# First products two units ahead of the second ones, w2's loads behind w1's, the second tile in halves, and a mixed last pair of units

## What is computed

```python
# x: [1536, 512] from the attention
logits = x @ w_gate                       # [1536, 8]
expert_idx = np.argmax(logits, axis=1)    # gate_w: softmax probability of that expert
for e in range(8):
    xe = x[expert_idx == e]
    h = np.maximum(xe @ w1[e], 0.0)       # w1[e]: [512, 1024]
    out[expert_idx == e] = gate_w * (h @ w2[e])   # w2[e]: [1024, 512]
h = out @ w_in                            # [512, 2048]
y = (h - np.tanh(h)) @ w_out              # [2048, 512]
```

## Time and profile before

| | us |
|---|---|
| median of 3 runs | 540.94 (538.23 to 541.13) |
| the profiled execution, its own time | 545.5 |
| its span, first to last instruction | 543.7 |
| TensorE busy | 516.3 (95%) |
| VectorE, ScalarE, GpSimd busy | 366.3, 262.3, 317.3 |
| mean granted clock of TensorE | 0.986 of 2.4 GHz |
| attention and routing | to about 73 |
| experts | about 73 to 270 |
| last stage and stores | about 270 to 543.7 |

### The profile page before, as it was taken

One profiled execution on the slowest core, in us unless ns is written; L12 is line 12 of the kernel. 1 busy time (PEld: TensorE's weight loads), 2 busy tenths in 40 slices (PEclk: granted clock), 3 DMA queues, 4 the chain that ended last, 5 costly groups with the idle time before them and its releaser, 6 DMA issues.

```text
span 543.7 us, 10934 instructions
## 1 busy us (share of the span) xinstructions
PE 516.3 (95%) x3974; PEld 458.5 (84%) x3975; DVE 366.3 (67%) x539; ACT 262.3 (48%) x484; POOL 317.3 (58%) x263
## 2 busy tenths in 40 slices
PE   5999959999899999999999999999999999999994
PEld 4999849999899999999878888888888888888883
DVE  7455444564436555365379999989997775997771
ACT  1244515655557666565455455545534444443431
POOL 4866056644344444454379898976855553875553
PEclk9999988999899999999999999999999999999998
DMA  8788636567576767766270000000100000100001
GB/s 321 249 287 287 202 115 186 205 196 204 181 222 203 230 184 224 243 184 214 89 276 1 1 1 1 1 1 25 54 1 1 0 1 1 59 20 2 0 1 77
DMA packets 32410, 64.56 MB, mean 119 GB/s; under 512 B 3696, under 2 KB 7792, under 8 KB 32368
## 3 DMA queue, kind: packets, MB, share of 16 engines
q1 hardware_dynamic: 30448, 57.71, 32.4%
q0 software_dynamic: 1920, 6.29, 3.5%
HBM read 57.69 MB, written 6.29 MB: 118 GB/s over the span
## 4 chain that ended last, share of the span: by engine, by line
PE 87%; DMA 4%; DVE 3%; issue 2%; ACT 2%; POOL 1%; SPq 1%; ACTq 0%; DVEq 0%; POOLq 0%
PE bank L315 26%; PE bank L317 25%; PE bank L316 25%; DMA wst<-in_w_dram 3%; PE bank L1129 2%; PE bank L1104 2%; PE bank L1115 2%; PE bank L1150 1%; PE bank L1212 1%; PE bank L1141 1%; PE bank L1157 1%; POOL out_dram L644 1%; DMA x_sorted<-token_rows,tokid 1%; ACT x_h L744 1%; PE bank L1287 1%
## 5 line engine op out<-in xcount | busy, mean ns | idle before, releaser
L603 POOL TENSOR_TENSOR w_l<-wst,w_h 128x512 fp32r<-128x512 f32 x64 | 84.0, 1313 | 93.6 <-ACT w_h L723 93.5
L652 POOL TENSOR_SCALAR big<-h_sq 128x512 uint8<-128x512 f32 x48 | 79.8, 1663 | 37.4 <-ACT h_sq L797 37.1
L665 POOL TENSOR_TENSOR g_l<-g,g_h 128x512 fp32r<-128x512 f32 x48 | 63.7, 1327 | 46.0 <-ACT g_h L807 46.0
L315 PE MATMUL bank<-xs_h,w_h 128*128 (+1 forms) x256 | 72.2, 282 | 4.2 <-DVE xs_l L1012 1.4
L315 PE MATMUL bank<-wo_h,g_h 128*128 128x512 f32 x192 | 75.4, 392 | 0.0
L317 PE MATMUL bank<-wo_l,g_h 128*128 128x512 f32 x192 | 75.1, 391 | 0.0
L316 PE MATMUL bank<-wo_h,g_l 128*128 128x512 f32 x192 | 74.6, 389 | 0.0
L317 PE MATMUL bank<-x_l,win_h 128*128 128x512 f32 x188 | 74.3, 395 | 0.0
L315 PE MATMUL bank<-h_h,w_h 128*128 128x232 f32 x256 | 71.9, 281 | 2.1 <-DVE h_l L1003 1.9
L315 PE MATMUL bank<-x_h,win_h 128*128 128x512 f32 x188 | 73.9, 393 | 0.0
L316 PE MATMUL bank<-x_h,win_l 128*128 128x512 f32 x188 | 73.7, 392 | 0.0
(11 more groups left out here) (146 smaller groups left out, 1111.0 us busy)
## 6 DMA issues: line engine op xcount, KB each, us to landing
wst<-in_w_dram SPq DMA_DIRECT2D x128, 256.0 KB, 3.1
qk_in<-in_qk_t_dram SPq DMA_DIRECT2D x12, 512.0 KB, 5.4
kv_in<-in_kv_dram SPq DMA_DIRECT2D x12, 512.0 KB, 4.5
win<-in_w_in_dram SPq DMA_DIRECT2D x8, 512.0 KB, 4.5
wo<-in_w_out_dram SPq DMA_DIRECT2D x8, 512.0 KB, 7.8
token_rows<-x_sb SPq DMA_DIRECT2D x12, 256.0 KB, 4.2
x_sorted<-token_rows,tokid POOLq DMA_INDIRECT x12, 4.3
out_dram<-rows,tokid POOLq DMA_INDIRECT x12, 3.1
```

The costliest lines, as they stand in the source:

```text
L315: pe.matmul(dst, lh, rh, start=start, stop=False, skip_group_check=True)
L603: pool.tensor_tensor(w2_l[:, j % STG], wst2[:, j % STG], w2_h[:, j % 2].bitcast(F32), ALU.subtract).then_inc(w2l_ready, 1)
L652: pool.tensor_scalar(big[:, f % 2], h_sq[:, f % 2], T * T, None, ALU.is_ge).then_inc(big_ready, 1)
L665: pool.tensor_tensor(g_l[:, f % 2], g[:, f % 2], g_h[:, f % 2].bitcast(F32), ALU.subtract).then_inc(gl_ready, 1)
```

## The change

It has four parts.

- TensorE's order in the experts: the first product of unit u+2 comes before the second product of unit u. Units 0 and 1 have their first products ahead of the loop. ScalarE and VectorE make w1's high and low part of unit u+3 in unit u's iteration; the high part has a wait of its own for the first product of unit u+1. `hidden` on ScalarE also waits for the second product of unit u-2, whose operand it overwrites. Tiles 2 to 11 are turned over six iterations of expert 0 in place of seven.
- SP's order: w2's load of unit u-2 stands behind w1's load of unit u.
- The second tile is transposed in two halves into two banks, with semaphores of their own, and the very first product waits for each half; ten keep-awake calls more (seven before the first tile, three between the tiles).
- The last two units of the last stage (46 and 47) are issued tile by tile in a mixed order, and their low parts of g are made on VectorE.

```diff
     LEAD = 6
     AHEAD = 3
+    W2_LATER = 2
     GATE_LAG = 3
     WP = F2 // E
+    LAST2 = NCH * FT - 2
...
     OV_STEPS = 20 + (E * OV - 1).bit_length()
-    LATER = [[t for t in range(2, NT) if (t - 2) * (JT - 1) // (NT - 2) == j] for j in range(JT)]
+    LATER = [[t for t in range(2, NT) if (t - 2) * (JT - 2) // (NT - 2) == j] for j in range(JT)]
     assert WIN <= 2 * P
...
         def tr_bank(t):
             return bank[:, 6 + t % 2, :].rearrange("p (k t) -> p k t", k=KT)
+        k_halves = [slice(0, KT // 2), slice(KT // 2, KT)]
+        tr_halves = [tr_bank(1)[:, k_halves[0]], bank[:, 5, :].rearrange("p (k t) -> p k t", k=KT)[:, k_halves[1]]]
...
                 load_kv(t)
-            def weights(src, j, unit, first):
+            def load_w1(src, j, unit, first=False):
                 if not first or j >= STG:
                     sp.wait_ge(first_done, unit - STG + 1)
                 sp.dma_start(wst1[:, j % STG].rearrange("p k f -> p (k f)"),
                              w1[src, j].rearrange("a p f -> p (a f)")).then_inc(w1_in[j % STG], 16)
+            def load_w2(src, j, unit, first=False):
                 if not first or j >= STG:
...
             def expert_loads(e, first=False):
                 for j in range(JT):
-                    weights(bass.ds(e, 1), j, JT * e + j, first)
+                    load_w1(bass.ds(e, 1), j, JT * e + j, first)
+                    if j >= W2_LATER:
+                        load_w2(bass.ds(e, 1), j - W2_LATER, JT * e + j - W2_LATER, first)
+                    elif not first:
+                        load_w2(bass.ds(e - 1, 1), JT + j - W2_LATER, JT * e + j - W2_LATER)
                     if j == 2:
...
             with sp.Fori(1, E) as e:
                 expert_loads(e)
+            for j in range(JT - W2_LATER, JT):
+                load_w2(bass.ds(E - 1, 1), j, JT * (E - 1) + j)
...
                     e = sp.value_load(ov_e[0:1, bass.ds(w, 1)], min_val=0, max_val=E - 1)
                     for j in range(JT):
-                        weights(bass.ds(e, 1), j, JT * E + JT * w + j, False)
+                        load_w1(bass.ds(e, 1), j, JT * E + JT * w + j)
+                        load_w2(bass.ds(e, 1), j, JT * E + JT * w + j)
                 sp.wait_ge(second_done, JT * (E + OV))
...
                     if unit + 1 < FT * NCH:
                         is_big((f + 1) % FT, unit + 1)
-                    pool.wait_ge(gh_ready, unit + 1)
-                    pool.tensor_tensor(g_l[:, f % 2], g[:, f % 2], g_h[:, f % 2].bitcast(F32),
-                                       ALU.subtract).then_inc(gl_ready, 1)
+                    if unit < LAST2:
+                        pool.wait_ge(gh_ready, unit + 1)
+                        pool.tensor_tensor(g_l[:, f % 2], g[:, f % 2], g_h[:, f % 2].bitcast(F32),
+                                           ALU.subtract).then_inc(gl_ready, 1)
                     if n and 1 <= f <= TPC:
...
             def hidden(j, unit):
                 act.wait_ge(first_done, unit + 1)
+                ge(act, second_done, unit - 1)
                 act.activation(h_h[:, j % 2], bank[:, j % 4, 0:WIN], ACT.Relu).then_inc(hh_ready, 1)
...
             def take(tiles):
                 for t in tiles:
-                    act.wait_ge(turned, t + 1)
+                    act.wait_ge(turned, max(t, 1))
                     act.copy(xs_h[:, :, t * P:(t + 1) * P], tr_bank(t)).then_inc(xsh_ready, 1)
-            take(range(2))
+            take(range(1))
+            for n, ks in enumerate(k_halves):
+                act.wait_ge(half_turned, n + 1)
+                act.copy(xs_h[:, ks, P:2 * P], tr_halves[n]).then_inc(half_high, 1)
...
                     unit = JT * e + j
                     hidden(j, unit)
-                    if not (last and j + 2 >= JT):
-                        w1_high(j + 2, unit + 2, arrived(e, j + 2))
+                    if not (last and j + 3 >= JT):
+                        act.wait_ge(first_done, unit + 2)
+                        w1_high(j + 3, unit + 3, arrived(e, j + 3))
                     if not (last and j + 1 >= JT):
...
                                  win[:, :, bass.ds(e * WP, WP)]).then_inc(winh_ready, 1)
+            act.wait_ge(first_done, 1)
+            w1_high(2, 2)
             n_ov = experts(act, expert)
...
             def take(tiles):
                 for t in tiles:
-                    dve.wait_ge(xsh_ready, t + 1)
+                    dve.wait_ge(xsh_ready, max(t, 1))
                     dve.tensor_tensor(xs_l[:, :, t * P:(t + 1) * P], tr_bank(t),
                                       xs_h[:, :, t * P:(t + 1) * P].bitcast(F32), ALU.subtract).then_inc(xsl_ready, 1)
-            take(range(2))
+            take(range(1))
+            for n, ks in enumerate(k_halves):
+                dve.wait_ge(half_high, n + 1)
+                dve.tensor_tensor(xs_l[:, ks, P:2 * P], tr_halves[n], xs_h[:, ks, P:2 * P].bitcast(F32),
+                                  ALU.subtract).then_inc(half_low, 1)
...
                     unit = JT * e + j
                     hidden(j, unit)
-                    if not (last and j + 2 >= JT):
-                        w1_low(j + 2, unit + 2)
+                    if not (last and j + 3 >= JT):
+                        w1_low(j + 3, unit + 3)
                     if first:
...
+            w1_low(2, 2)
             n_ov = experts(dve, expert)
...
             dve.wait_ge(y_high_ready, E)
+            def g_low(f, unit):
+                dve.wait_ge(gh_ready, unit + 1)
+                dve.tensor_tensor(g_l[:, f % 2], g[:, f % 2], g_h[:, f % 2].bitcast(F32),
+                                  ALU.subtract).then_inc(gl_last, 1)
             def less_tanh(f, unit):
...
                 dve.wait_ge(quad_used, unit + 1)
                 dve.scalar_tensor_tensor(gf, gf, POLY_C, uf, ALU.mult, ALU.mult).then_inc(poly_step, 1)
+                if unit == LAST2 + 1:
+                    g_low(f - 1, unit - 1)
                 dve.wait_ge(big_ready, unit + 1)
...
                     if f == 0 and n:
                         outputs(n - 1)
+            g_low(FT - 1, LAST2 + 1)
             outputs(NCH - 1)
...
                 i = pe.matmul(psId, in_row[:, t], ids[:, t], start=t == 0, stop=t == NT - 1)
             i.then_inc(id_done, 1)
-            keep_awake(pe, 13)
+            keep_awake(pe, 20)
...
                 for t in tiles:
                     pe.wait_ge(gathered[t], 16)
-                    ge(pe, xsl_ready, t - 1)
+                    ge(pe, xsl_ready, t - 2)
                     for k in range(KT):
...
                     i.then_inc(turned, 1)
-            def first_product(off, j, unit):
+            def turn_in_halves(t):
+                pe.wait_ge(gathered[t], 16)
+                for k in range(KT):
+                    i = pe.transpose(tr_halves[k // (KT // 2)][:, k % (KT // 2)], x_sorted[:, t, k * P:(k + 1) * P], ident[:])
+                    if k % (KT // 2) == KT // 2 - 1:
+                        i.then_inc(half_turned, 1)
+            def first_product(off, j, unit, by_halves=False):
...
                 pe.wait_ge(w1l_ready, unit + 1)
                 for k in range(KT):
+                    if by_halves and k % (KT // 2) == 0:
+                        pe.wait_ge(half_low, k // (KT // 2) + 1)
                     i = three(pe, bank[:, j % 4, 0:WIN], w1_h[:, j % 2, k, :], w1_l[:, j % STG, k, :],
...
                 off = offset(e)
                 for j in range(JT):
-                    if j + 1 < JT:
-                        first_product(off, j + 1, JT * e + j + 1)
+                    if j + 2 < JT:
+                        first_product(off, j + 2, JT * e + j + 2)
                     elif not last:
-                        if first:
-                            pe.wait_ge(xsl_ready, NT)
-                            pe.wait_ge(pad_ready, 2)
-                        first_product(offset(e + 1), 0, JT * e + JT)
+                        if j + 2 == JT:
+                            if first:
+                                pe.wait_ge(xsl_ready, NT - 1)
+                                pe.wait_ge(pad_ready, 2)
+                            off = offset(e + 1)
+                        first_product(off, j + 2 - JT, JT * e + j + 2)
                     if j == 0 and not first:
...
             pe.wait_ge(ov_step, 2)
-            turn(range(2))
-            pe.wait_ge(xsl_ready, 2)
-            first_product(0, 0, 0)
+            turn(range(1))
+            keep_awake(pe, 3)
+            turn_in_halves(1)
+            pe.wait_ge(xsl_ready, 1)
+            first_product(0, 0, 0, by_halves=True)
+            first_product(0, 1, 1)
...
                 i.then_inc(hidden_done, 1)
+            def tile2(i, f):
+                sl = slice(i * P, (i + 1) * P)
+                return three(pe, bank[:, 4 + i, :], g_h[:, f % 2, sl], g_l[:, f % 2, sl], wo_h[:, f], wo_l[:, f],
+                             f == 0, f == FT - 1)
+            def last_outputs():
```

(19 more changed lines are left out.)

## The result

The changed kernel takes 538.17 us (median of 20 runs, 536.56 to 540.25), the kernel before 541.37 (20 runs on the same chips, 538.23 to 543.88). The ratio is 0.9944, 95% interval 0.9929 to 0.9958: 3.2 us or 0.56% faster (interval 2.3 to 3.8 us), so close to the 0.5% bound that the interval lies across it. Forecast was 539.5, range 534.3 to 543.0. The profiled execution after took 537.62, span 535.8.

A forecast was written before the change was run, and what follows sets the result against it. TensorE, 87% of the span, was taken as the bound. 3.0 - 2.5 - 1.7 + 4.0 + 2.8 - 0.8 + 1.0 = 5.8 us off the profiled 545.5 gave 539.7; 1.5 off the median 540.94 gave 539.4; forecast 539.5, range 534.3 to 543.

The forecast's parts named there:

- Halves: Experts' start: the second tile passing in halves starts the first product of unit 0 earlier, 1.2 us won (0.6 to 1.4).
- The clock: Experts' start: ten more keep-awake calls and the earlier first product hold full clock, 2.1 us won (0 to 2.1).
- F(2): First product of unit 2, experts' start: waits for w1's high part, made after unit 0's first product, 0.3 us lost.
- Rival 2: Experts' start: the clock falls all the same, filling too thin; 2.1 us not won, 541.6; chance 0.20.
- F(11): First product of unit 11, expert 1: waits 3.7 us for w1 behind `win`; low clock after it costs 1.7.
- w1(11)'s landing: Load of w1 for unit 11, behind expert 1's `win`: lands 5.3 us after issue; 4.1 to 6.4 in other experts.
- Rival 1: Expert 0 to 1: F(11) does not wait, so 3.7 + 1.7 are not lost: 534.1; chance 0.15.
- expert 2's 4.0 us: Old order, expert 2: waits of 1.4, 0.8 and 0.1 plus 1.7 for low clock, won; timed runs thought mostly without them.
- S(63): Second product of unit 63, end of expert 7: waits for w2's low part from GpSimd, 0.8 us lost.
- the tail: End of the last stage: tile 0 done 1.36 us earlier, g's low part 0.35 late, 1.0 us won.
- Rival 3: Timed runs have expert 2's wait as profiled: the full 5.8 us comes off the median, 535.1; chance 0.13.
- Rival 4: Experts behind `win`: ScalarE stops for w1 ahead of w2; each of six experts loses 1.0, 545.5; chance 0.10.

The follow-up runs named there:

- without the tail: Changed kernel with the tail as before (units 46 and 47 in order, g's low parts on GpSimd): 539.12 us, ratio 0.9969 to the kernel before.
- w2 one later: Changed kernel with w2's load one unit behind w1's instead of two: 538.63 us, ratio 0.9953 to the kernel before.
- w2 beside w1: Changed kernel with w2's load right behind w1's of the same unit, new TensorE order kept: 565.15 us, ratio 1.0438 to the kernel before.
- the early split: Changed kernel with expert 0's win split at j = 3, not 7: 533.7 us; plus S(61) ahead of F(63): 532.89; plus offset read before the waits: 531.78.
- keep-awake as before: Changed kernel with the old 13 keep-awake calls and none between the tiles: 540.15 us, ratio 0.9961 to the kernel before.
- the second profile: The kernel before, unchanged, profiled once more: one run, 542.63 us, span 540.9.
- start and tail: Changed kernel with the experts' order, loads and splits put back as before; halves, ten keep-awake calls and mixed tail stay: 538.15 us, ratio 0.9918.
- the order alone: Changed kernel with start and tail put back as before, the new TensorE and SP order kept: 540.79 us, ratio 0.9995 to the kernel before.

## Why the prediction was right or wrong

**Start: right in both parts, together somewhat smaller.** Halves were taken as 1.2 us, measured 1.06 from the transposes to F(0) (1.16 with the filling ahead). The clock was taken as held, 2.1 won; it is held, and worth 1.6 to 1.9 in the old order (25.91 against 27.49 and 27.84 from F(0) to F(8)) and 1.1 to 1.5 in the new. The rest goes into F(2)'s wait: 0.3 foretold, 0.44 to 0.47 in six profiles (without the tail, w2 one later, w2 beside w1, and the three with the early split), 0.92 in that of the changed kernel, where ScalarE started 0.50 us after what released it. With matmuls at half rate that wait is hidden: the two profiles in the new order without the ten calls have none. Rival 2, the clock falls anyway, is refuted.

**Expert 0 to 1: the mechanism right, the term too large.** F(11) lost 2.66 where 3.7 was taken (bounds 3.0 to 5.3). The mis-sized term is w1(11)'s landing: I took the row of this place, 5.3, and rows of other experts, 4.1 to 6.4, and it landed in 3.8 (109.40 to 113.16). That is not luck of one execution: in the six profiles with the new order and the late split it lands in 3.6 to 3.8, and F(11) is 2.58 to 2.76 late. In the old order it takes 3.6, 3.8 and 4.1 in the three other profiles, so the 5.3 that I took is the one row that stands apart. The sentence on the Trainium skill (DMA: Bandwidth & Descriptors, Bandwidth), by which the estimate was a landing of 3.5 and a wait of 2.4, was nearer than my rows. What makes a landing of 5.3 was not tried. That a wait of this length drops the clock for one stretch came out, 0.50 for 3.4 us behind it, in four of the six, and for 6.8 in a fifth (keep-awake as before). In the sixth (w2 beside w1) F(11) is 2.76 late, TensorE busy for 0.80 of 3.40 us, and the clock stays at 1.00: the drop is likely after such a wait, not certain. Rival 1 is refuted as a forecast, but its saving is real: the early split brings it.

**Experts 2 to 7: the gaps right, what the timed runs have of them too small.** All gaps are gone. I wrote that the timed runs "mostly lack" 4.3 us of the profiled ones, which leaves 3.7 in experts 1 to 7 (1.2 in expert 1 and 2.8 in experts 3 to 7, less 0.3). Of expert 2's 4.0 us, 1.7 recur in the second profile. The two profiles near their medians have 4.5 and no low clock, so the step is 0.8 short; by the mean of all four, 5.4 and 0.4 for the clock, it is 2.1 short. Which of the two holds for the timed runs four profiles cannot tell.

**The sum.** In the order of the prediction: 1.1 for the halves, 2.1 for the clock, 0.45 off for F(2), 2.7 and 1.7 off for F(11) and its clock, 4.5 for the old gaps, 0.9 off for S(63), 0.9 for the tail: 2.8 us (4.1 by the mean of all four profiles), beside 3.2 measured, interval 2.3 to 3.8. The forecast for the timed runs was 1.5. Of the 1.3 between, F(11)'s size is 1.0 and the gaps 0.8; the start takes 0.3 of it back and S(63) and the tail 0.2. Rival 3, all of 5.8, is refuted. The predicted 539.5 against 538.17 has the sign and the mechanisms right, but the gain is twice the 1.5 forecast, for those two terms; the range held a loss of 2 us and a gain of 7, so to lie in it says little. It calls "same" likeliest, and the measured 0.56% lies just beyond that bound.

**The order as a whole.** In the timed terms I had it lose 2.8 (2.5 + 1.7 + 0.8 + 0.3 of F(2), less 2.5 of gaps that remain), and start and tail win 4.3. Measured: start and tail 4.4 won; the order alone 0.3 won, with an interval from 1.4 won to 0.8 lost. The product of the two ratios is 0.9913, and the whole change has 0.9944; of the 0.3% between, 1.7 us, F(2)'s wait, which is only there with both, is 0.45 to 0.92; the intervals are wider than the rest, and what it is is not shown. Start and tail came out as forecast; the order alone was priced 3 us too low (2.0 to 4.2 by the interval), of which the same two terms are 1.8 and F(2) 0.3.

**S(63) and tail: right.** 0.88 for 0.8; 0.86 for 1.0, of it 0.35 late at the low part of g as worked out.

**Rival 4, a stop in each expert, is refuted** for this kernel: ScalarE had its w1 in time everywhere but in expert 1. The run with w2 beside w1 shows the same stop where SP has less lead, at up to 3.4 us an expert.

In the two profiled executions 0.7 us of the 7.9, in the experts, is in no gap over 0.12 us. The rows place it: behind a product that starts late, at full clock the second matmul starts 0.18 to 0.21 us after the first in place of 0.11 (before, 166.62 and 166.80), so each gap costs 0.07 to 0.10 more than its size. From F(8) on the kernel before has sixteen gaps, the changed one three, and F(2). The prediction's sum leaves this out.

## What to carry to other kernels

When products are moved ahead, list for each load the instruction that frees its buffer and everything ahead of it in the issuing queue: here one rare split, placed late for expert 0 where it cost nothing, held a whole queue and gave back all that the new order had won. Before pricing waits off one profile, take a second one of the same kernel: half of its largest gap in the experts was in that execution alone, and so was the landing of 5.3 us where 3.6 came again. And look at what fixed order an engine's own waits impose on cheap steps: a register read moved over two waits took 0.76 us off F(8).

## What was not expected of the hardware

A w1 load of 256 KB behind `win` of 512 KB landed in 3.6 to 6.4 us in different places and runs: 3.6, 3.8, 4.1 and 5.3 for w1(11) in the old order, 3.6 to 3.8 in the new one with the late split, 4.2 with the early one, and 4.1, 4.5 and 6.4 in other experts. One row is a poor price for it. ScalarE started 0.50 us after the matmul that released it in one profile; in six others F(2) came 0.44 to 0.47 late in all. And TensorE at 1.66 busy of 3.40 us was followed by a low clock in one execution, while the second profiled execution of the same kernel, with waits of 0.58 and 0.63 in the same place and 2.18 busy of 3.40 (139.0 to 142.4), kept it. Nor does the length of the wait alone decide: with w2 beside w1, a wait of 2.76 us left the clock at 1.00 and one of 2.13 was followed by a low one.
